# Window attention and two feed-forward layers: inputs turned by VectorE and moved within SBUF by DMA, in place of TensorE's transposes

## The reference

```python
w = softmax(weight_gen, axis=-1)                       # per token and head
out[b, s, h, :] = sum_k w[b, s, h, k] * x_pad[b, s + k, h, :]   # 7 taps, x padded by 6 rows of zeros
x1 = out.reshape(8192, 192)
h = x1 @ w_in1                # 192 -> 2048
y = (h * cos(h)) @ w_out1     # 2048 -> 192
h2 = y @ w_in2
result = maximum(0.01 * h2, h2) @ w_out2
```

## Time and profile before

| | |
|---|---|
| median of 3 runs | 1160.34 us (1159.18 to 1161.13) |
| profiled execution, its own time | 1158.45 us |
| span of the profiled execution, first to last instruction | 1156.7 us |
| mean granted TensorE clock | 0.999 of 2.4 GHz |
| TensorE matmuls (PE) busy | 1137.8 us (98%) |
| TensorE weight loads (PEld) busy | 956.0 us (83%) |
| VectorE (DVE) busy | 915.1 us (79%) |
| ScalarE (ACT) busy | 723.9 us (63%) |
| GpSimd (POOL) busy | 84.8 us (7%) |

### The profile page before, as it was taken

How to read it: one execution, slowest core, us unless ns; L and a number is a source line. 1 busy time by engine, 2 the same in 40 slices (tenths; PEclk the granted TensorE clock), 3 DMA queues, 4 the chain that set the end, 5 groups by cost and what they waited for, 6 DMA issues and landing times.

```text
span 1156.7 us, 23276 instructions
## 1 busy us (share of the span) xinstructions
PE 1137.8 (98%) x9990; PEld 956.0 (83%) x9990; DVE 915.1 (79%) x892; ACT 723.9 (63%) x774; POOL 84.8 (7%) x81
## 2 busy tenths in 40 slices
PE   7899999999999999999999999999999999999998
PEld 5678888888888888888888888888888898889976
DVE  8888797878889788797787878878797787978433
ACT  5666674766657576575755747566575665757544
POOL 5860000000000000000000000000000000000000
PEclk9999999999999999999999999999999999999999
DMA  9660100101001010100101001010100101000001
GB/s 260 200 126 1 35 1 8 43 1 49 1 14 37 1 49 1 49 1 6 44 2 49 1 11 39 1 49 1 26 25 3 47 1 49 1 9 7 1 15 28
DMA packets 70334, 37.41 MB, mean 32 GB/s; under 512 B 56796, under 2 KB 66394, under 8 KB 69848
## 3 DMA queue, kind: packets, MB, share of 16 engines
q1 hardware_dynamic: 65784, 30.68, 10.4%
q0 software_dynamic: 4448, 5.24, 2.5%
HBM read 29.61 MB, written 6.29 MB: 31 GB/s over the span
## 4 chain that ended last, share of the span: by engine, by line
PE 88%; DVE 4%; ACT 3%; SPq 2%; POOL 2%; issue 1%; DMA 1%; ACTq 0%; POOLq 0%
PE slot L1100 41%; PE acc_a L1100 27%; PE acc_b L1100 18%; DVE g_lo L848 2%; DVE prods L309 1%; DMA x_win<-in_x 1%; ACT gate L726 1%; POOL prods L309 1%; ACT g_hi L661 1%; POOL prods L300 1%; SPq L467 0%; DVE prods L300 0%; POOL out_hi_lo L578 0%; ACT L781 0%; ACT L786 0%
## 5 line engine op out<-in xcount | busy, mean ns | idle before, releaser
L1100 PE MATMUL acc_a<-g_hi,out_hi_lo 64*128 64x512 f32 x2000 | 696.3, 388 | 0.0
L1100 PEld LDWEIGHTS acc_a<-g_hi,out_hi_lo 64*128 64x128 f32 x2000 | 367.8, 184 | 34.5 <-issue 0.5
L848 DVE TENSOR_TENSOR g_lo<-gate,g_hi 128x1024 fp32r<-128x1024 f32 x248 | 304.1, 1227 | 108.6 <-ACT g_hi L661 108.1
L1100 PE MATMUL acc_b<-g_hi,out_hi_lo 64*128 64x512 f32 x1000 | 388.3, 388 | 1.5 <-DVE g_lo L848 1.2
L1100 PE MATMUL acc_a<-g_lo,out_hi_lo 64*128 64x512 f32 x1000 | 386.6, 387 | 0.0
L1100 PE MATMUL acc_b<-g_lo,out_hi_lo 64*128 64x512 f32 x1000 | 386.5, 387 | 0.0
L661 ACT ACTIVATE g_hi<-gate 128x1024 fp32r<-128x1024 f32 x248 | 262.8, 1060 | 98.9 <-PE acc_b L1100 81.8
L1100 PE MATMUL slot<-x_a_hi,in_a_lo 64*128 64x512 f32 x1024 | 299.3, 391 | 3.8 <-DVE g_lo L839 2.4
L1100 PE MATMUL slot<-x_b,in_b_hi 64*128 64x512 f32 x1024 | 297.1, 387 | 0.2 <-DVE x_b L862 0.2
L1100 PE MATMUL slot<-x_a_lo,in_a_hi 64*128 64x512 f32 x1024 | 297.0, 387 | 0.0
L1100 PE MATMUL slot<-x_a_hi,in_a_hi 64*128 64x512 f32 x1024 | 296.9, 386 | 0.0
(11 more groups left out here) (102 smaller groups left out, 1056.8 us busy)
## 6 DMA issues: line engine op xcount, KB each, us to landing
x_win<-in_x SPq DMA_DIRECT2D x14, 960.0 KB, 4.9
out<-turned_a SPq DMA_DIRECT2D x240, 16.0 KB, 1.5
out<-turned_b SPq DMA_DIRECT2D x120, 16.0 KB, 1.5
out_raw<-in_moe_w_out SPq DMA_DIRECT2D x3, 512.0 KB, 8.4
out_hi_lo<-in_moe_w_out POOLq DMA_DIRECT2D x2, 768.0 KB, 11.0
out_hi_lo<-in_moe_w_out POOLq DMA_DIRECT2D x1, 1536.0 KB, 14.5
taps_w<-in_weight_gen SPq DMA_DIRECT2D x2, 560.0 KB, 9.5
in_a_raw<-in_moe_w_in SPq DMA_DIRECT2D x1, 1024.0 KB, 5.1
```

The source lines that it names most:

```text
L848: nc.vector.tensor_tensor(g_lo[:, q % 2, :], result_of(i - b, q), g_hi[:, q % 2, :].bitcast(FP32), ALU.subtract)\
L1100: return nc.tensor.matmul(to, w[rows, :], x[rows, :], start=start, stop=stop)
```

## The change

From chunk 2 on, TensorE's 16 transposes per chunk are gone. In step 13 VectorE transposes the finished attention of the chunk, `prods` 0, in blocks of 32 x 32 into `prods` 1 (`turn_input`, one instruction over 768 columns). SyncE's queue then moves the blocks between partitions with 24 DMAs from SBUF to SBUF (`move_input`: 6 groups of 32 features by 4 groups of 32 partitions, each 32 rows of 512 bytes), into a new tile `x_raw_a` and a part of `result`. ScalarE and VectorE make the high and low parts from there, in step 16 in place of step 15. In SyncE's order the moves of chunk i + 1 stand ahead of `store(i - 2)` and `load_x(i + 2)`. The columns of a chunk stand in another order now, so the stores and the reads of the accumulators have other access patterns, of the same sizes.

At the start chunk 1's last product (tap 0) goes from GpSimd to VectorE, into a place of its own; GpSimd does `out_lows(2)` before its first addition; only three units of iteration 0 stay in PSUM; the last four parts of the softmax of chunk 1 and of chunk 2 are done apart, chunk 2's in step 9; VectorE's last two additions for chunk 1 move to step 6, and the low parts of its input stand behind that step's first instruction. The chunks 0 and 1 keep TensorE's transposes.

```diff
+TURN_INPUT_STEP = 13
...
-        if step == (FIRST_INPUT_STEP if i == 0 else INPUT_STEP):
-            return "input" if i <= C - 2 else None
+        if i == 0 and step == FIRST_INPUT_STEP:
+            return "input"
...
-        return i == 0 and q < len(FIRST_UNITS)
+        return i == 0 and q in (2, 3, 4)
...
+        x_raw_a = sb("x_raw_a", [P, N])
...
-        ATT_DVE, ATT_POOL, ATT_END = 2, 9, 5
+        ATT_DVE, ATT_POOL, ATT_END = 2, 8, 5
...
-        SOFT_CHUNKS = [(0, 1), (1, 3), (3, 6), (6, 11), (11, C)]
+        SOFT_HEADS = [(0, 1), (1, 3), (3, 6), (6, 11), (11, C)]
+        SOFT_CHUNKS = [(0, 1), (1, 2), (2, 3), (3, 6), (6, 11), (11, C)]
...
-                    engine.wait_ge(filled, fills(c - 2, INPUT_STEP) if c > 1 else 1)
+                    if c <= 2:
+                        engine.wait_ge(filled, fills(0, INPUT_STEP) if c == 2 else 1)
+                    else:
+                        engine.wait_ge(x_moved, MOVES * (c - 2))
...
+            if c == 1:
+                yield lambda: product(0, APART, 0, J).then_inc(apart, 1)
+                yield lambda: after(8, lambda: add(0, 0, 1))
+                yield lambda: after(9, add_apart)
+                return
...
+            def move_input(c):
+                if c > 2:
+                    sp.wait_ge(x1_ready, 2 * c)
+                sp.wait_ge(x_turned, c - 1)
+                for n, d in enumerate(range(0, dim, BLOCK)):
+                    to = x_raw_a[d:d + BLOCK, :] if d < DA else x_raw_b[d - DA:d - DA + BLOCK, :]
+                    for k in range(P // BLOCK):
+                        sp.dma_start(to[:, k * P:(k + 1) * P],
+                                     prods[k * BLOCK:(k + 1) * BLOCK, 1, n * P:(n + 1) * P])\
+                            .then_inc(x_moved, 16)
...
+            move_input(2)
             load_x(3)
...
+            for i in range(2, C - 1):
+                move_input(i + 1)
                 store(i - 2)
-                load_x(i + 2)
...
             out_lows(1)
-            of_pool[2]()
             out_lows(2)
-            for instruction in of_pool[3:]:
+            for instruction in of_pool[2:]:
                 instruction()
...
             def split_high(i, step, chunk):
+                if chunk >= 2:
+                    act.wait_ge(x_moved, MOVES * (chunk - 1))
+                    nc.scalar.activation(x1_a_hi[:, :], x_raw_a[:, :], ACT.Copy).then_inc(x1_hi, 1)
+                    nc.scalar.activation(x1_b[0:DB, :], x_raw_b, ACT.Copy).then_inc(x1_hi, 1)
...
-                if step == INPUT_STEP - 1 and input_splits(i, INPUT_STEP):
+                if step == INPUT_STEP and input_splits(i, INPUT_STEP):
                     split_high(i, INPUT_STEP, i + 1)
...
+            def turn_input(c):
+                dve.wait_ge(att, (c + 1) * ATT_STEPS)
+                nc.vector.transpose(prods[:, 1, :],
+                                    prods[:, 0, :].rearrange("p (j d r) -> p d j r", j=J, r=BLOCK))\
+                    .then_inc(x_turned, 1)
...
+                if step == TURN_INPUT_STEP and 1 <= i <= C - 2:
+                    turn_input(i + 1)
                 if step == TURN_STEP and i >= 2:
                     turn_result(i)
...
-            def rest_of_iteration(i, q):
-
-                after = UNITS[q] + 1
-                if after == INPUT_STEP and kind(i, after) == "input":
-                    both_products(i, q, i, q - LAG, lambda: wait_for_input(i, INPUT_STEP))
-                    transpose_input(slots[INPUT_STEP % SLOTS])
-                else:
-                    both_products(i, q, i, q - LAG)
```

More of the change, by code:

```diff
@@ L94, in input_splits @@
             return step == FIRST_INPUT_SPLIT
-        return kind(i, step) == "input"
+        return step == INPUT_STEP and i <= C - 2
     def first_out(i, step):
@@ L236, in window_attention_two_ffn @@
         clock_ready = sem("clock_ready")
+        apart = sem("apart")
         soft = sem("soft")
@@ L401, in first_lows @@
                    b_pairs(W1.in_b_hi, cols).bitcast(FP32))
-        EXP_STEP, SINE_STEP = 10, 14
-        SOFT_ROWS = [slice(a * J * heads, b * J * heads) for a, b in SOFT_CHUNKS]
-        SOFT_AT = {}
+        EXP_STEP, SINE_STEP = 10, 12
+        HEAD_ROWS, SOFT_ROWS = [[slice(a * J * heads, b * J * heads) for a, b in chunks]
+                                for chunks in (SOFT_HEADS, SOFT_CHUNKS)]
+        SOFT_AT = {(0, 9): [(2, part) for part in TAIL_PARTS]}
         for n, (begin, end) in enumerate(((1, 1), (2, 3), (4, 5)), 2):
@@ L526, in _ @@
             load_gen(4)
+            move_input(2)
             load_x(3)
-            store(0)
-            load_x(4)
-            for i in range(3, C - 2):
+            for i in range(2, C - 1):
+                move_input(i + 1)
                 store(i - 2)
-                load_x(i + 2)
-            for c in range(C - 4, C - 1):
+                if i + 2 < C:
+                    load_x(i + 2)
+            for c in range(C - 3, C - 1):
                 store(c)
@@ L669, in split_high @@
             def split_high(i, step, chunk):
[L671 to L676, removed]
+                if chunk >= 2:
+                    act.wait_ge(x_moved, MOVES * (chunk - 1))
+                    nc.scalar.activation(x1_a_hi[:, :], x_raw_a[:, :], ACT.Copy).then_inc(x1_hi, 1)
+                    nc.scalar.activation(x1_b[0:DB, :], x_raw_b, ACT.Copy).then_inc(x1_hi, 1)
+                else:
+                    act.wait_ge(filled, fills(i, step))
+                    slot = slots[step % SLOTS]
+                    nc.scalar.activation(halves(x1_a_hi[:, :]), slot[:, :, 0:N // 2], ACT.Copy)\
+                        .then_inc(x1_hi, 1)
+                    nc.scalar.activation(halves(x1_b[0:DB, :]), slot[0:DB, :, N // 2:N], ACT.Copy)\
+                        .then_inc(x1_hi, 1)
                 if chunk <= 2:
@@ L933, in step_of @@
                         .then_inc(fraction, 1)
+                if step == FIRST_INPUT_SPLIT and input_splits(i, step):
+                    split_low(FIRST_INPUT_STEP, i + 1)
+                if (i, step) == (0, ATT_END + 1):
+                    for instruction in of_chunk_1[ATT_POOL + 1:]:
+                        instruction()
                 pending_low(i, step)
@@ L970, in softmax @@
             def softmax(n, part):
-                rows = SOFT_ROWS[n]
+                rows = (HEAD_ROWS if part in HEAD_PARTS else SOFT_ROWS)[n]
                 weights, sums = taps_w[:, rows, :], scratch[:, rows]
@@ L989, in softmax @@
                     dve.wait_ge(soft, soft_count(n, "invert"))
-                    ins = nc.vector.tensor_tensor(*softmax_operands(n), ALU.mult)
+                    ins = nc.vector.tensor_tensor(*softmax_operands(rows), ALU.mult)
                 ins.then_inc(soft, 1)
-            for part in SOFT_PARTS:
+            for part in HEAD_PARTS + TAIL_PARTS:
                 softmax(0, part)
@@ L1031, in transpose_input @@
                         rows = slice(k * DB, (k + 1) * DB)
-                        nc.tensor.transpose(slot[:, k, j * DB:(j + 1) * DB],
+                        nc.tensor.transpose(columns(slot[:, k, 0:N // 2])[:, j],
                                             prods[rows, 0, j * dim:j * dim + DA], ident[rows, rows])
```

116 lines of the change are left out of this document (69 added, 47 removed).

## The result

The changed kernel takes 1375.62 us in the median (1373.26 to 1376.97, 4 runs), the kernel before 1159.83 us beside it: a ratio of 1.186, with a 95% interval of 1.1844 to 1.1872. It is slower by 216 us. Its time lies 84 us above the forecast of 1292 us, and above the range's upper end of 1340 us.

What follows compares the result with a forecast made beforehand. TensorE was taken to bound the kernel. Per chunk 7.2 (longer period) + 0.9 (low parts) + 1.7 (clock) = 9.8 us; 14 chunks 137 us, less 5 at the start, on 1158.45: 1290, by the median 1292 us; range 1221 to 1340.

Steps and rivals of the forecast that it cites:

- what bounds the kernel: Whole kernel: TensorE, busy 98% of the span, sets the time; any wait in its stream costs its full length.
- 24 issues in a row on one queue: SyncE's queue, turn to next fill of unit 0: hiding them would need 0.13 us from one issue to the next.
- the turn: VectorE, step 13: transposing 768 columns takes 1.00 us, in a place where VectorE sits idle 2.55 us.
- stores and loads behind the moves: SyncE's queue: a chunk's stores and `load_x`, issued after the moves, are covered by most of a period.
- the step on SyncE's queue: The 24 moves: 0.465 us from issue to issue, bounds 0.36 and 0.50, so the last issues 10.7 us after the first.
- rival 3: SyncE's queue: the moves are hidden and the kernel is faster, 1148 us; chance 0.05.
- slow rival (2): Moves are slower than stores, or the clock costs twice as much: 13.5 us per chunk, 1344 us; chance 0.10.
- the landing: After the last move's issue: its data lands 1.5 us later, with bounds 1.4 and 2.3 us.
- the clock and the low parts: TensorE, each chunk: 1.7 us lost to a lowered clock, 0.9 us waiting for VectorE's low parts.
- The start: First 60 us: the new order of work for chunk 1 gains 5 us, between 2 and 7.
- The worth of the removed transposes: TensorE, chunks 2 to 15: a block of transposes costs about 0.54 us, 7.6 us at most over 14 times.
- The rule: DMA issue on a queue: initiating is usually small beside the DMA itself; by it alone the time would be 1148 us.

Runs made afterwards that it cites:

- e7: The kernel before plus seven bursts of DMAs behind all its work: 591 to 601 ns per issue within SBUF, 421 to 432 ns with one end in DRAM.
- e11: The changed kernel with 57 matmuls that nothing reads filling TensorE's pause in iterations 2 to 15: 1356.82 us, ratio 1.1710.
- e1: The changed kernel with chunks 2 to 15 back on TensorE's transposes, the new start kept: 1157.57 us, ratio 0.9979 to the kernel before.
- e2: The changed kernel with 2 large moves per chunk in place of 24, all bytes copied but blocks not brought to their places: 1158.99 us.
- e4: The changed kernel with the 24 moves shared out, 12 on SyncE's queue and 12 on ScalarE's: 1277.63 us.
- e5: The changed kernel with the 24 moves shared out, 12 on SyncE's queue and 12 on GpSimd's: 1270.58 us.
- e12: The changed kernel with the 24 moves shared out, 8 each on SyncE's, GpSimd's and ScalarE's queues: 1249.41 us.
- e8: The changed kernel with the turned input sent through DRAM, 4 stores and 2 loads per chunk in place of 24 moves: 1241.78 us.
- e3: The changed kernel with 12 moves of twice the length per chunk, same bytes but blocks not brought to their places: 1271.08 us.
- e6: The changed kernel with 50 matmuls that nothing reads put into TensorE's pause in iterations 2 to 15: 1371.87 us.

## Why the prediction was wrong

**Right:** what bounds the kernel, and that a wait put into TensorE's stream costs its full length; that 24 issues in a row on one queue can't fit between the turn and unit 0 of the next iteration; that TensorE is released from the wait by ScalarE's high part, 14 times; that the turn costs 1.00 us (0.97 measured); that the clock falls at each pause; that stores and loads behind the moves cost nothing (in these chunks no engine is seen waiting for one of them).

**Failed: the step on SyncE's queue.** It took 0.465 us from issue to issue from the stores, "same size of DMA, same queue, same kind of burst". What it took as equal, the kind of the two ends, is what decides: 0.64 us with both in SBUF (e7). The row of the upper bound, 0.50 us, was also one with an end in DRAM, so the bound could not hold the truth. The prediction did say that no row shows a DMA from SBUF to SBUF, but it let that count for the quick side alone (rival 3); its slow rival (2) stayed at the stores' 0.505 us. Fewer and longer runs, from which it expected cheaper moves, change nothing in e7. From the first issue to the restart this gives 17.3 us in the mean in place of 12.8, so 4.5 us per chunk: 0.17 x 23 = 4.0 us for the issues, 0.3 us for the landing (1.8 against 1.5 us), and some tenths.

**Mis-sized: the clock and the low parts.** They were 1.7 + 0.9 = 2.6 us in the forecast. From the restart at 655.59 to the next first issue at 723.31 are 67.7 us, where 64.0 was the distance before: 3.7 us here, and 4.0 us in the mean (68.1), so 1.4 us more than forecast. The low stretch reached 6.4 us behind the restart, not the 3.5 us of the earlier trace rows, and so lost 3.2 us of full clock in this chunk; it had begun in the pause. The waits for the low parts lie largely inside it, so the two terms don't simply add: without the low clock 1.6 of the 4.0 us remain (e11). The upper bound of 3.4 + 1.3 us held.

Together: 9.8 us were forecast per chunk. With 4.5 us more on SyncE's queue and 1.4 us more for the clock and the low parts this is 15.7 us, which is what came (85.4 - 69.7), and 14 x 15.7 = 220 us.

**The start** was forecast to give 5 us, between 2 and 7; e1 shows 2.4 to 2.9 us. The size was taken too high, inside its bounds. The additions were indeed done about as soon as forecast, the pause of 2.54 us and the low clock of the earlier trace rows are gone, but the period of chunk 2 gave part of it back: the low part of the input began 0.74 us sooner in chunk 1 (57.35 against 58.09 us) and 3.65 us sooner in chunk 2 (125.89 against 129.54), and by chunk 15 the lead is 2.64 us (1033.04 against 1035.68).

**The worth of the removed transposes** (0.54 us per chunk, the third rival's gain) was not collected even where the wait was gone (e2): the split in step 16 spends about half of it, and the iterations with softmax the rest. So the third rival's 1148 us was out of reach for this placement at any price of an issue.

**The rule** of the Trainium skill that was weighed (DMA: Bandwidth & Descriptors, "Issuing engines are not separate DMA queues"), that the time to initiate a DMA is usually small beside the DMA, does not hold here: one issue takes 0.59 us beside 1.8 to the landing, and 24 in a row take 15.3 us. The other half of the same sentence, that DMAs started from several engines save the initiating time, agrees with e4, e5 and e12: 98 to 126 us less.

The time after the moves are shared follows the count of issues on the longest queue: 24 gave 1376 us, 12 gave 1271 to 1278, 8 gave 1249. The last step is smaller: 4 issues fewer would be 2.5 us, and from the first issue to the restart e12 takes 8.5 us where e5 took 9.8. In e12 the last moves are mostly ScalarE's, which begin 1.1 us after SyncE's, and each lands 0.4 us later. The price behind the restart hardly depends on the pause: the restart to the next first issue takes 67.6 to 68.1 us in the mean with pauses of 2.9 us (e8) up to 12.4 us, where it was 64.0 us before.

Not settled: what in the issue of a DMA with both ends in SBUF takes the 0.17 us more. A version with the attention a whole iteration ahead, which would hide any of these transfers, was not tried; the transposes that it would take out are worth 7.6 us at most, and e2 collected none of them.

## What to carry to other kernels

Count DMA issues, not bytes, when a transfer has to fit into a gap: many small DMAs in a row cost the queue 0.4 to 0.6 us each before the last one even starts. Look for a price of the same kind in both ends (SBUF to SBUF is not SBUF to DRAM) before a row is borrowed, and if there is none, let the upper bound reach well beyond the borrowed row. Where TensorE is saturated, taking 0.5 us of work out of it is soon lost again: in this kernel a wait of 2.9 us per chunk (e8) cost another 3 us behind it.

## What the hardware showed that had not been expected

- An issue from SyncE's queue took 591 to 601 ns with both ends in SBUF and 421 to 432 ns with one end in DRAM, whatever the rows, runs and quarters (e7). GpSimd issued the same moves in 0.49 us each (e5).
- SyncE's queue kept its 0.64 us per move while ScalarE's issued such DMAs at 0.63 us (e4). With three queues at work the moves landed after 2.2 us in place of 1.8 us (e12).
- Pauses of 2.9 and 3.6 us in the mean brought the granted clock down to a mean of 0.966 and 0.968 (e8, e12), not far from the 0.956 of pauses of 4.9 us (e3). In e8 it fell behind a pause of 2.05 us and stayed up behind one of 2.03 us. In e6 it fell behind pauses of 1.3, 0.5 and 0.5 us.
- With fillers on TensorE the 24 moves took 0.4 to 0.5 us longer to issue in the mean (e6, e11). The median issue stayed at 591 ns, but 11 and 12 of 336 issues took over 0.7 us, where 4 did in the changed kernel. That the fillers are the cause is not shown.
